# A chunked linear-attention and two-MLP kernel: moving a state's decay and four products to ScalarE, with new orders for the first unit

## The reference, cut to what matters

```python
B, H, S, D = 4, 8, 768, 48                       # r, k, v: (B, H, S, D)
for t in range(S):                               # attention with a decaying state
    cur = u * kt (outer) vt
    y[:, :, t] = rt @ (state + cur)
    state = w[None, :, :, None] * state + kt (outer) vt
x = y as (B, S, H * D)                           # 4 x 768 x 384
h = relu(x @ w_in)                               # 384 -> 1024
conv_out = 3-tap convolution of h along the sequence, per channel
x = (h * sigmoid(conv_out)) @ w_out              # 1024 -> 384
xn = (x - mean) / sqrt(var + 1e-6) * g_ln
out = x + relu(xn @ w_ch1) @ w_ch2               # 384 -> 1536 -> 384
```

## Time and profile before

| | |
|---|---|
| median of 3 executions | 639.19 us (639.11 to 639.89) |
| the profiled execution | 639.75 us, its span 637.5 us |
| PE busy | 615.8 us, 97% of the span |
| PEld busy | 558.9 us, 88% |
| DVE busy | 424.8 us, 67% |
| ACT busy | 260.4 us, 41% |
| POOL busy | 133.0 us, 21% |
| granted TensorE clock | 1.000 |
| chain that ended last | PE 91%, DVE 4%, issue, DMA, ACT and POOL 1% each |
| DMA | 38.8 MB, HBM 60 GB/s over the span |

### The profile page before, as it was taken

The page is one execution under the profiler, slowest core; times in us unless marked ns, Lnnn a source line. Parts: engine busy times, 40 slices in busy tenths (PEclk is TensorE's granted clock), DMA queues, the critical chain, the costliest instruction groups (busy, mean ns, idle before and its releaser), DMA issues.

```text
span 637.5 us, 10898 instructions
## 1 busy us (share of the span) xinstructions
PE 615.8 (97%) x4434; PEld 558.9 (88%) x4434; DVE 424.8 (67%) x689; ACT 260.4 (41%) x466; POOL 133.0 (21%) x139
## 2 busy tenths in 40 slices
PE   2899999999999999999999999999999999999997
PEld 2787989999998999999999989989999999989996
DVE  7899986798556686555885556865649754376343
ACT  1266644364333264331743423643316534165330
POOL 4741054300432102421003321033010031000200
PEclk9999999999999999999999999999999999999999
DMA  8980230211302311101022023121110100010001
GB/s 216 317 282 30 88 101 16 67 43 32 101 1 67 110 30 61 44 30 52 30 66 69 0 68 108 30 67 39 44 66 7 61 1 1 1 43 1 0 1 42
DMA packets 15200, 38.78 MB, mean 61 GB/s; under 512 B 2096, under 2 KB 8112, under 8 KB 15152
## 3 DMA queue, kind: packets, MB, share of 16 engines
q1 hardware_dynamic: 15152, 38.10, 19.1%
HBM read 33.37 MB, written 4.72 MB: 60 GB/s over the span
## 4 chain that ended last, share of the span: by engine, by line
PE 91%; DVE 4%; issue 1%; DMA 1%; ACT 1%; POOL 1%; SPq 0%; DVEq 0%; POOLq 0%
PE hid L396 14%; PE acc L396 13%; PE hid L397 13%; PE hid L398 13%; PE acc L398 13%; PE acc L397 13%; PE att_ps L410 3%; PE att_ps L450 3%; PE att_ps L445 2%; PE att_ps L424 1%; PE att_ps L457 1%; DMA raw_n<-rk_n 1%; PE acc L544 1%; PE hid L410 0%; DVE w_raw L701 0%
## 5 line engine op out<-in xcount | busy, mean ns | idle before, releaser
L396 PE MATMUL acc<-ring_hi,w_hi 128*128 128x440 f32 (+1 forms) x420 | 153.6, 366 | 0.3 <-DVE ring_lo L790 0.3
L398 PE MATMUL acc<-ring_hi,w_lo 128*128 128x440 f32 (+1 forms) x420 | 151.8, 361 | 0.0
L397 PE MATMUL acc<-ring_lo,w_hi 128*128 128x440 f32 (+1 forms) x420 | 151.4, 360 | 0.0
L623 ACT ACTIVATE ring_hi<-hid 128x440 fp32r<-128x440 f32 (+1 forms) x84 | 45.1, 536 | 178.8 <-PE hid L398 176.4
L827 DVE SCALAR_TENSOR_TENSOR ring_lo<-hid,ring_hi 128x440 fp32r<-128x440 f32 (+1 forms) x84 | 50.8, 611 | 92.9 <-ACT ring_hi L623 92.9
L396 PE MATMUL hid<-x_hi,w_hi 128*128 128x440 f32 (+1 forms) x252 | 94.6, 375 | 0.5 <-DVE ring_lo L827 0.3
L397 PE MATMUL hid<-x_lo,w_hi 128*128 128x440 f32 (+1 forms) x252 | 91.5, 363 | 0.0
L398 PE MATMUL hid<-x_hi,w_lo 128*128 128x440 f32 (+1 forms) x252 | 91.2, 362 | 0.0
L396 PEld LDWEIGHTS acc<-ring_hi,w_hi 128*128 128x128 f32 x420 | 78.9, 188 | 6.4 <-issue 0.6
L398 PEld LDWEIGHTS acc<-ring_hi,w_lo 128*128 128x128 f32 x420 | 78.8, 188 | 5.2
L397 PEld LDWEIGHTS acc<-ring_lo,w_hi 128*128 128x128 f32 x420 | 78.9, 188 | 4.7
(11 more groups left out here) (128 smaller groups left out, 950.6 us busy)
## 6 DMA issues: line engine op xcount, KB each, us to landing
rk<-rk_t SPq DMA_DIRECT2D x22, 448.0 KB, 3.6
raw_n<-rk_n SPq DMA_DIRECT2D x22, 384.0 KB, 3.7
w_raw<-weights SPq DMA_DIRECT2D x10, 768.0 KB, 14.6
v_sb<-v_n SPq DMA_DIRECT2D x22, 192.0 KB, 2.4
out<-x SPq DMA_DIRECT2D x18, 220.0 KB, 2.2
first_rk<-rk_t SPq DMA_DIRECT2D x2, 448.0 KB, 11.3
first_raw_n<-rk_n SPq DMA_DIRECT2D x2, 384.0 KB, 11.5
out<-x SPq DMA_DIRECT2D x3, 218.0 KB, 2.1
```

What stands on the lines that cost most here:

```text
L396: mm(ps, lh, rh, start=start, stop=False)
L397: mm(ps, lh, rl, start=False, stop=False)
L398: return mm(ps, ll, rh, start=False, stop=stop)
L623: nc.scalar.activation(ring_hi[:, tile % RING, 0:n], hid[f % 2][:, 0:n], ACT.Relu).then_inc(act_hi, 1)
```

## The change

**State.** The table is multiplied by w to the 128th before it is transposed: ACT makes four copies of `powk` with a per-partition factor into `att` (free at that time), and PE transposes `att`; it waits for those copies instead of for DVE's tables. So `kd` and `kv` hold the factor already. DVE's `state` becomes two operations in place of three (one addition per half; for the first chunk of a row a copy). The decay of the old state is a new ACT step `decay`: four copies of 112x96 with a per-partition factor into the other state buffer, which need the old state and the `y` of the chunk before; `state` then adds in place. There are 16 decays: 4 in each batch row (4 in the first lists, 12 later).

**Values times dots.** `cv` of chunks 0 to 3 is made on ACT, with 8 copies of 128x48 with a per-partition factor; later chunks keep POOL's. `dots` and `x_sum` wait for ACT's count in those chunks.

**First weight piece.** `w_low 0` is made in two halves of 768 columns; `mm1 0` and `mm1 1` need the first, `mm1 2` the second.

**Orders.** All five lists up to the end of the first unit are new. SP issues the small loads `w` and `const` ahead of the first large one. PE makes `scores 1` before `kv 0`, and `kv 2` after `y 2`. The step `table`, at the end of `ACT_FIRST` before, stands after `relu 3` of unit 0. In the plans of later units only `decay` is new.

```diff
-    ("scores", 0), ("kv", 0), ("scores", 1), ("y", 0), ("kv", 1), ("scores", 2), ("xt", 0), ("y", 1), ("kv", 2),
-    ("xt", 1), ("scores", 3), ("y", 2), ("y", 3), ("kv", 3), ("xt", 2), ("xt", 3), ("means", 0), ("mm1", 0),
+    ("scores", 0), ("scores", 1), ("kv", 0), ("y", 0), ("scores", 2), ("kv", 1), ("xt", 0), ("y", 1), ("xt", 1),
+    ("scores", 3), ("y", 2), ("kv", 2), ("y", 3), ("xt", 2), ("kv", 3), ("xt", 3), ("means", 0), ("mm1", 0),
...
 ACT_FIRST = [
-    ("xh", 0), ("xh", 1), ("w_hi", 0), ("xh", 2), ("xh", 3), ("w_hi", 1), ("mean", 0), ("relu", 0), ("relu", 1),
...
-    ("fhi", 8), ("sum_hi", 1), ("fhi", 9), ("fhi", 10), ("root",), ("fhi", 11), ("table",), ("xh", 6)]
+    ("cv", 0), ("decay", 1), ("cv", 1), ("xh", 0), ("decay", 2), ("xh", 1), ("cv", 2), ("w_hi", 0), ("cv", 3),
+    ("xh", 2), ("xh", 3), ("decay", 3), ("w_hi", 1), ("relu", 0), ("relu", 1), ("relu", 2), ("sig", 0),
+    ("relu", 3), ("table",), ("mean", 0), ("sig", 1), ("hi", 0), ("w_hi", 2), ("hi", 1), ("relu", 4), ("sig", 2),
...
+    ("square", 2), ("fhi", 8), ("sum_hi", 1), ("fhi", 9), ("fhi", 10), ("root",), ("fhi", 11), ("xh", 6)]
 ACT_PLAN = [
-    ("relu", 0), ("relu", 1), ("sig", 0), ("hi", 0), ("relu", 2), ("sig", 1),
+    ("decay", 0), ("relu", 0), ("relu", 1), ("sig", 0), ("hi", 0), ("relu", 2), ("sig", 1),
...
-    ("sig", 7), ("hi", 6), ("hi", 7), ("xh", 0),
+    ("sig", 7), ("hi", 6), ("hi", 7), ("decay", 1), ("xh", 0),
...
-    ("fhi", 0), ("fhi", 1), ("xh", 1), ("sum_hi", 0), ("fhi", 2), ("fhi", 3), ("fhi", 4),
+    ("fhi", 0), ("fhi", 1), ("decay", 2), ("xh", 1), ("sum_hi", 0), ("fhi", 2), ("fhi", 3), ("fhi", 4),
...
 DVE_FIRST = [
-    ("scale", 0), ("powkt",), ("scale", 1), ("dots", 0), ("masked", 0, 0), ("masked", 0, 1), ("state", 0),
-    ("masked", 1, 0), ("masked", 1, 1), ("scale", 2), ("state", 1), ("dots", 1), ("x_sum", 0), ("masked", 2, 0),
-    ("scale", 3), ("dots", 2), ("x_sum", 1), ("x_low", 0), ("state", 2), ("masked", 2, 1), ("x_low", 1),
-    ("masked", 3, 0), ("masked", 3, 1), ("dots", 3), ("x_sum", 2), ("x_sum", 3), ("w_low", 0), ("x_low", 2),
-    ("x_low", 3), ("state", 3), ("scale", 4), ("w_low", 1), ("conv", 0), ("dots", 4), ("conv", 1), ("gated", 0),
+    ("scale", 0), ("powkt",), ("dots", 0), ("scale", 1), ("scale", 2), ("masked", 0, 0), ("masked", 0, 1),
+    ("masked", 1, 0), ("state", 0), ("dots", 1), ("masked", 1, 1), ("x_sum", 0), ("scale", 3), ("state", 1),
+    ("masked", 2, 0), ("x_sum", 1), ("dots", 2), ("masked", 2, 1), ("x_low", 0), ("masked", 3, 0),
+    ("masked", 3, 1), ("x_low", 1), ("dots", 3), ("state", 2), ("w_low", 0, 0), ("x_sum", 2), ("x_sum", 3),
+    ("x_low", 2), ("w_low", 0, 1), ("x_low", 3), ("state", 3), ("scale", 4), ("w_low", 1), ("conv", 0),
...
 POOL_FIRST = [
-    ("ruk", 0), ("kd", 0), ("ruk", 1), ("kd", 1), ("cv", 0), ("ruk", 2), ("cv", 1), ("kd", 2), ("ruk", 3),
-    ("kd", 3), ("pad",), ("cv", 2), ("cv", 3), ("ruk", 4), ("cv", 4), ("kd", 4), ("ruk", 5), ("cv", 5),
+    ("ruk", 0), ("kd", 0), ("ruk", 1), ("kd", 1), ("ruk", 2), ("kd", 2), ("ruk", 3), ("kd", 3), ("ruk", 4),
...
 SP_FIRST = [
-    ("load_t", 0), ("small", "w"), ("small", "const"), ("small", "u"), ("load_n", 0), ("load_t", 1), ("load_n", 1),
-    ("load_v", 0), ("load_t", 2), ("small", "g"), ("load_v", 1), ("load_n", 2), ("load_v", 2), ("load_t", 3),
-    ("load_n", 3), ("load_w", "in0"), ("load_v", 3), ("load_w", "c1_0"), ("small", "cw"), ("load_w", "in1"),
+    ("small", "w"), ("small", "const"), ("load_t", 0), ("small", "u"), ("load_n", 0), ("load_v", 0),
+    ("small", "g"), ("load_t", 1), ("load_t", 2), ("load_n", 1), ("load_n", 2), ("load_t", 3), ("load_v", 1),
+    ("load_v", 2), ("load_n", 3), ("load_v", 3), ("load_w", "in0"), ("load_w", "c1_0"), ("small", "cw"),
...
-            pe.wait_ge(dve_pow, POW_STEPS)
+            pe.wait_ge(act_tab, 1)
...
+            def cv(m):
+                act.wait_ge(dve_red, m + 1)
+                loaded(act, m, 2)
+                for h in range(H):
+                    cols = slice(h * D, (h + 1) * D)
+                    last = copy(raw_n_of(m)[:, 0, cols], v_of(m)[:, cols], scale=c8[:, h:h + 1])
+                last.then_inc(act_cv, 1)
+
+            def decay(m):
...
+                old, behind = state[m % 2], state[(m + 1) % 2]
+                act.wait_ge(dve_st, states_made(m - 1))
+                act.wait_ge(pe_y, m)
+                for hp in range(NP):
+                    last = copy(behind[0:ROWS, hp, :], old[0:ROWS, hp, :], scale=w_pow[0:ROWS, 7, hp:hp + 1])
+                last.then_inc(act_dec, 1)
...
+            act.wait_ge(dve_pow, POW_STEPS + 1)
+            for hp in range(NP):
+                last = copy(att[:, hp, :], powk[:, hp, :], scale=w_pow[:, 7, hp:hp + 1])
+            last.then_inc(act_tab, 1)
...
                     if c == 0:
-                        last = tt(behind[rows, :, cols], new, w128(rows, D), ALU.mult)
+                        last = nc.vector.tensor_copy(behind[rows, :, cols], new)
                     else:
-                        last = tt(behind[rows, :, cols], new, old[rows, :, cols], ALU.add)
-                if c:
-                    last.then_inc(dve_add, 1)
-                    dve.wait_ge(dve_add, 4 * (m // CH) + c)
-                    rows = slice(0, ROWS)
-                    last = tt(behind[rows, :, :], behind[rows, :, :], w128(rows, 2 * D), ALU.mult)
+                        last = tt(behind[rows, :, cols], new, behind[rows, :, cols], ALU.add)
```

More of the change, by code:

```diff
@@ L114 @@
[L114 to L123, removed]
@@ new lines @@
+    ("x_low", 2), ("w_low", 0, 1), ("x_low", 3), ("state", 3), ("scale", 4), ("w_low", 1), ("conv", 0),
+    ("conv", 1), ("conv", 2), ("gated", 0), ("conv", 3), ("gated", 1), ("low", 0), ("dots", 4), ("low", 1),
+    ("masked", 4, 0), ("masked", 4, 1), ("gated", 2), ("conv", 4), ("gated", 3), ("low", 2), ("w_low", 2),
+    ("x_sum", 4), ("scale", 5), ("state", 4), ("gated", 4), ("conv", 5), ("conv", 6), ("low", 3), ("gated", 5),
+    ("w_low", 3), ("conv", 7), ("low", 4), ("gated", 6), ("gated", 7), ("low", 5), ("low", 6), ("low", 7),
@@ new lines @@
+    ("centre", 0), ("dots", 5), ("masked", 5, 0), ("masked", 5, 1), ("x_low", 4), ("x2_low", 0), ("w_low", 4),
+    ("x2_low", 1), ("x2_low", 2), ("w_low", 5), ("flow", 0), ("flow", 1), ("centre", 1), ("flow", 2), ("w_low", 6),
+    ("scale", 6), ("flow", 3), ("x_sum", 5), ("centre", 2), ("sum_low", 0), ("w_low", 7), ("x_low", 5),
+    ("masked", 6, 0), ("flow", 4), ("w_low", 8), ("flow", 5), ("scale", 7), ("off_mean", 0), ("w_low", 9),
+    ("flow", 6), ("off_mean", 1), ("off_mean", 2), ("flow", 7), ("flow", 8), ("sum_low", 1), ("flow", 9),
@@ L125 @@
+    ("masked", 6, 1), ("variance",), ("dots", 6), ("x_sum", 6), ("flow", 10), ("state", 6), ("flow", 11),
+    ("dots", 7), ("newton",), ("x_low", 6), ("scaled", 0), ("result", 0), ("scaled", 1), ("result", 1),
+    ("scaled", 2), ("result", 2)]
 DVE_PLAN = [
@@ L139 @@
 POOL_FIRST = [
[3 rows of a table removed]
+    ("ruk", 0), ("kd", 0), ("ruk", 1), ("kd", 1), ("ruk", 2), ("kd", 2), ("ruk", 3), ("kd", 3), ("ruk", 4),
+    ("cv", 4), ("kd", 4), ("ruk", 5), ("cv", 5), ("sums", 0), ("sums", 1), ("ruk", 6), ("pad",), ("cv", 6),
+    ("kd", 6), ("ruk", 7), ("kd", 7), ("cv", 7)]
 POOL_PLAN = [
@@ L336, in loaded, with valued @@
                 eng.wait_ge((ld_t, ld_n, ld_v)[what][m % 2], 16 * ((m - AHEAD) // 2 + 1))
+        def valued(eng, m):
+            if m < AHEAD:
+                eng.wait_ge(act_cv, m + 1)
+            else:
+                eng.wait_ge(pool_cv, m + 1 - AHEAD)
         piece = lambda name: slice(PIECE_AT[name], PIECE_AT[name] + PIECE)
@@ L466, in mm1 @@
             def mm1(u, f):
-                if f % 4 == 0:
-                    piece_whole(u, f"in{f // 4}")
+                if u == 0 and f == 0:
+                    pe.wait_ge(lo_first, 1)
+                elif u == 0 and f == 2:
+                    piece_whole(u, "in0")
+                elif f == 4:
+                    piece_whole(u, "in1")
                 if f == 0:
@@ L474, in mm1 @@
                     pe.wait_ge(act_relu, F1 * u + f - 1)
[L475 removed]
+                t = slice(0, N_OF[u] + 2)
                 for k in range(KT):
                     cols = first_cols("in", f, k)
[L478 to L479 removed]
+                    last = split_product(hid[f % 2][:, t], w_hi[:, cols], w_lo[:, cols],
+                                         xt_hi[u % 2][:, k, t], xt_lo[u % 2][:, k, t], k == 0, k == KT - 1)
                 last.then_inc(pe_hid, 1)
@@ L654, in _ @@
                 "table": table, "root": root, "sum_hi": sum_high, "relu": relu, "sig": sigmoid, "hi": hi, "fhi": fhi, "x2": keep_x2, "x2_hi": x2_high,
-                "square": square, "xh": xh, "w_hi": w_high, "mean": column_mean}, ACT_FIRST)
+                "square": square, "xh": xh, "decay": decay, "cv": cv, "w_hi": w_high, "mean": column_mean}, ACT_FIRST)
         @block.vector
@@ L690, in _ @@
```

(18 more changed lines are left out.)

42 lines of the change are left out of this document (21 added, 21 removed), and 15 rows, old and new, of tables (PE_FIRST, POOL_FIRST).

## The result

The changed kernel takes 634.97 us (median of 4, 634.05 to 635.57) against 639.38: ratio 0.9929, interval 0.9912 to 0.9946. The profiled execution took 635.06 us, its span is 633.3.

The account below looks back on a forecast made before the run. TensorE, busy 615.75 of 637.5 us, was taken to bound the kernel, its idle time being what can be won. 0.8 (start) + 1.0 (later units) - 0.1 (table) = 1.7 us gained, giving 637.5 us; range 635.4 to 639.4.

Parts of the forecast that it names:

- the walk: Working through the five engine lists up to mm1 0: it starts at 36.9 in place of 37.68, 0.8 us gained.
- the rise: TensorE's matmuls going from half to full speed (1.2 to 2.4 GHz) in unit 0, taken to lie near 26 us.
- rival B: Start: TensorE reaches full speed at 20 in place of 26, mm1 0 2.05 us earlier, 635.45 us; chance 0.14.
- the rest of unit 0: TensorE's idle 0.59 us in unit 0 after mm1 0 starts: no change, bounds 0.4 us either way.
- the later units: Two TensorE waits for DVE's scale shrink from 0.9 to 0.4 us: 1.0 us gained, less 0.1 for the table load.
- Small load: Start: w, ahead of the first large load, lands at 3.4; tables come 1.2 us earlier, worth nothing.
- cv on ACT: Chunks 0 to 3: eight copies take 1.9 us on ACT, bounds 1.2 and 2.6; POOL loses 0.87 us each.
- rival C: Unit 0: ScalarE's chain binds if cv costs over 1.9 us, mm1 0 1.2 us later, 638.7 us; chance 0.22.
- Decay: State step: DVE loses 0.56 us per state, ACT gains four copies of 1.2 us, bounds 0.7 and 1.3.
- Rival E: Later units: state waits for ACT's decay, so the two 0.9 us waits stay, 638.5 us; chance 0.12.
- the halves: First half of w_low 0 runs before x_sum 2 and 3 in 0.95 us, removing x_low 3's delay of mm1 0.
- The missing table step: Unit 1: a 1.28 us Sigmoid table load delays its first sigmoid and relu 2; 0.1 us lost, bounds 0 and 0.8.

Follow-up runs that it names:

- before_again: The kernel before, unchanged, run once more: 640.68 us in its one execution.
- new_ops_old_orders: The changed kernel with the five old lists, decays put into ACT's, cv on POOL, w_low 0 whole: 638.85 us against 639.66 for the kernel before.
- before_fill: The kernel before with 2 matmuls on zeros behind scores 0, in the gap before kv 0: 639.04 us against 639.66 without them.
- after_wlow_whole: The changed kernel with w_low 0 in one operation at the second half's place: 635.17 us against 640.37 for the kernel before.
- after_state_dve: The changed kernel with the decay from chunk 4 on back on DVE, none on ACT: 636.9 us against 640.37 for the kernel before.
- after_fill_table: The changed kernel with 2 matmuls on zeros behind scores 0 and the table step back behind root: 634.80 us against 634.79 for the changed kernel.
- after_gap: The changed kernel with TensorE's scores 2 also waiting for x_sum 0, a gap of about 1 us: 637.75 us against 639.95 for the kernel before.

## Why the prediction was wrong, point by point

**The step that failed** is "with these durations, and TensorE slow up to 26.1, I went through the five lists". TensorE was slow up to 20.3 only, and mm1 0 came at 34.42, not at 36.9. The rest of the walk held: with the rise at 20 it gives 36.9 - 2.05 = 34.85, and raw_n 0 landed half a microsecond earlier than I took (ruk 0 ran from 9.71), which is worth some tenths. That was rival B, at 0.14. By parts, from the two profiles: mm1 0 gained 3.26 us where 0.8 was forecast, the rest of unit 0 0.53 where nothing was, the later units 0.70 where 0.9 was, and 0.3 was lost at the end.

Rival B was given 0.14 because of the argument "before, TensorE was busy without much of a gap from 14.56 on, and still slow at 20.38". As a reading it is right, and before_again makes it stronger: slow at 20.41 without any gap from 15.0 to 22.5. What did not follow is that the new order must be slow as long. Its price was worked out, its chance was not, and the central walk assumed one place of the rise for both kernels without a reason.

Why the rise comes earlier is known in part. From one group of kernels to the next, fewer or shorter gaps went with an earlier rise; within a group it scatters by up to 2.7 us and does not follow them. The changed kernel and its variants with no gap over 0.3 us from about 14 on rose at 18.4 to 20.5 (6 profiles); with the gap before scores 1 filled too, near 16 (2 profiles); with 0.93 us at 16, at 22.4; with 1.05 us at 19.1, later than 34. With the old start it rose at 26.0 to 28.7 (3 profiles); with a shorter gap before kv 0 at 19.6 (new_ops_old_orders), with that gap filled at 17.8 (before_fill). But gaps do not explain all of it: before_again had 2.2 us idle before 15.0, then 7.5 us without a gap, and stayed slow; after_wlow_whole had 2.25 us idle before 14.5 and rose at 19.2, with one gap of 0.26 us. What separates these two stays open. It is not the place in a list alone, since new_ops_old_orders rose early in the old lists.

**Small load.** w's table step ran at 3.00, earlier than the 3.4 taken. That is outside the bound of 3.2. Alone it is worth 0.3 us in the profile; nothing was forecast.

**cv on ACT.** 1.91 us against 1.9 forecast. It did not bind (rival C): x_sum 3 started at 30.55, when y 3 was done, and cv 3 had ended at 30.0. The overlap of 65 ns in its lower bound stands in no row.

**Decay.** 1.17 us against 1.2. The two waits shrank to 0.4 us each, 1.0 us in total, as forecast; after_state_dve and new_ops_old_orders show that it is the decay's place that does it. Rival E fell for these two waits. What it feared, a decay in another engine's way, did happen with the old lists: mm1 4 of unit 1 in new_ops_old_orders.

**w_low in halves.** The first half ran in the idle place, 0.96 us. But the halves were credited with removing x_low 3's delay, and after_wlow_whole keeps the gain without them. By the timeline x_low 2 now stands ahead of the piece, and TensorE's means 0 covers the rest; in that run no POOL instruction held the piece, which depends on when the load that ruk 4 waits for lands.

**Rest of unit 0.** Forecast zero, bounds 0.4; 0.53 us was won, a little outside. TensorE had no idle time there, against 0.59, most of it one wait of 0.3 us for DVE's L827 and one of 0.2 us before a y.

**The missing table step.** mm1 4 of unit 1 came 0.15 us later against mm1 0 than before (8.69 to 8.54 us), mm1 5 0.25 us later (12.40 to 12.15); 0.1 was forecast. after_fill_table, with the step back, has 8.54 and 12.14 again, so it is the step that does it.

**The orders as a whole.** The new operations in the old lists gave 0.8 us in the median, which is not apart from the noise, and 1.2 us at the last matmul of the profile; the rest of the 4.4 to 4.9 us comes with the new lists. The filled gap alone gave 0.6 us (before_fill), the lists with a late rise about 2.2 (after_gap, its own gap included). Neither alone gives the whole, and how much of it belongs to each is not separated further.

## What to carry to other kernels

When a start-up phase runs its matmuls at half speed, ask of a new order not only what waits it removes but whether it leaves the matmuls in one run: one gap of 1 us cost 2.2 to 2.7, itself included. Walk the lists twice, with the speed's rise early and late, and give the two ends the chances. Work that fills a wait on which nothing hangs (kv 0 behind scores 1) was still worth 1 us, because full speed came earlier.
